# First pair of an attention kernel: low queries of head A on GpSimd, and maxima of four tiles from high halves alone

## The reference

```python
scores = scale * matmul(rotate(q), rotate(k).T)
attn = exp(scores - max(scores)); attn = attn / (sum(attn) + 1e-9)
x = (attn @ v), heads side by side          # 2304 x 512
h = x @ w_in                                # 2304 x 1024
solu = h * softmax(h)
out = layer_norm(solu) * g_ln @ w_out       # 2304 x 512
```

## Time and profile before

| | |
|---|---|
| median of 3 runs | 483.8 us (483.62 to 483.8) |
| the profiled execution | 483.53 us |
| its span | 481.8 us |
| PE busy | 473.4 us (98%) |
| DVE, ACT, POOL busy | 381.4, 250.4, 236.1 us |

### The profile page before, as it was taken

How to read it: one execution, slowest core, us unless ns; L and a number is a source line. 1 busy time by engine, 2 the same in 40 slices (tenths; PEclk the granted TensorE clock), 3 DMA queues, 4 the chain that set the end, 5 groups by cost and what they waited for, 6 DMA issues and landing times.

```text
span 481.8 us, 7983 instructions
## 1 busy us (share of the span) xinstructions
PE 473.4 (98%) x2553; PEld 402.9 (84%) x2553; DVE 381.4 (79%) x591; ACT 250.4 (52%) x397; POOL 236.1 (49%) x307
## 2 busy tenths in 40 slices
PE   7899999999999999999999999999999999999997
PEld 7678888988898889888888878888888888888885
DVE  6867898889889888988896366999897899888731
ACT  4667677777777777777777352032223222322221
POOL 6877666867686768667772021342352121222110
PEclk9999999999999999999999999999999999999999
DMA  8503544645455545445424203233333233322242
GB/s 295 188 12 77 151 147 113 184 131 168 101 156 164 161 116 152 145 123 169 135 71 100 68 6 59 34 83 69 85 87 62 51 51 68 80 57 60 59 81 84
DMA packets 101009, 50.61 MB, mean 105 GB/s; under 512 B 90280, under 2 KB 90280, under 8 KB 99048
## 3 DMA queue, kind: packets, MB, share of 16 engines
q1 hardware_dynamic: 100152, 50.00, 38.7%
q10 hardware_dynamic: 816, 0.10, 0.1%
HBM read 33.33 MB, written 4.79 MB: 79 GB/s over the span
## 4 chain that ended last, share of the span: by engine, by line
PE 95%; DVE 2%; ACT 1%; DMA 1%; issue 0%; SPq 0%; DVEq 0%; ACTq 0%
PE ps L1169 20%; PE ps L1183 20%; PE ps L1155 20%; PE ps L1106 18%; PE ps L1077 8%; PE ps L1135 4%; PE ps L1121 4%; DMA X<-x_in 1%; DVE nm L843 1%; DVE X L780 1%; DVE QK L816 0%; DVE X L785 0%; ACT QK L595 0%; ACT p_main L650 0%; ACT QK L610 0%
## 5 line engine op out<-in xcount | busy, mean ns | idle before, releaser
L843 DVE TENSOR_REDUCE nm<-ps 128x1 fp32r<-128x576 f32 x144 | 108.1, 755 | 31.7 <-PE ps L1077 29.1
L1155 PE MATMUL ps<-p_main,V 128*128 128x288 f32 x404 | 114.8, 406 | 0.0
L1169 PE MATMUL ps<-w_hi,KB 128*128 128x512 f32 x288 | 91.5, 390 | 0.0
L1183 PE MATMUL ps<-w_hi,QK 128*128 128x512 f32 x288 | 91.0, 389 | 0.0
L1106 PE MATMUL ps<-QK 128*128 128x288 f32 x320 | 90.0, 362 | 0.8 <-ACT p_main L650 0.5
L650 ACT ACTIVATE p_main<-ps 128x576 f32<-128x576 f32 x101 | 65.7, 651 | 42.6 <-PE ps L1106 41.2
L1155 PEld LDWEIGHTS ps<-p_main,V 128*128 128x128 f32 x404 | 71.0, 190 | 10.8 <-ACT p_main L650 0.2
L412 POOL TENSOR_TENSOR X<-X,rope 128x1152 f32<-128x1152 f32 x26 | 68.5, 2660 | 10.8 <-POOL v_lo_b L453 8.2
L1106 PEld LDWEIGHTS ps<-QK 128*128 128x128 f32 x320 | 55.6, 189 | 17.9 <-issue 5.7
L1106 PE MATMUL ps<-KB 128*128 128x288 f32 x320 | 67.8, 293 | 0.0
L486 POOL COPY V<-oe 32x256 f32<-32x256 f32 x72 | 29.8, 413 | 74.2 <-DVE QK L894 41.6
(11 more groups left out here) (118 smaller groups left out, 717.8 us busy)
## 6 DMA issues: line engine op xcount, KB each, us to landing
X<-x_in SPq DMA_DIRECT2D x13, 1152.0 KB, 5.1
V<-oe SPq DMA_DIRECT2D x213, 32.0 KB, 1.9
V<-v_in SPq DMA_DIRECT2D x32, 160.0 KB, 2.8
out<-X SPq DMA_DIRECT2D x18, 256.0 KB, 2.3
w_raw<-w_in SPq DMA_DIRECT2D x16, 256.0 KB, 2.9
xT<-x_in SPq DMA_DIRECT2D x2, 1152.0 KB, 10.2
xT<-oe SPq DMA_DIRECT2D x16, 144.0 KB, 2.4
inv<-inv_rows SPq DMA_DIRECT2D x16, 144.0 KB, 3.0
```

The costliest lines, as they stand in the source:

```text
L843: nc.vector.tensor_reduce(nm[g][:, at:at + 1], src[:, :, 0:HALF], AX_XY, ALU.max, negate=True)\
L1155: ins = nc.tensor.matmul(o_ps[a][:, half, 0:HALF], v, p[:, half * HALF:(half + 1) * HALF], start=(k == 0), stop=(k == 9))
L1169: ins = nc.tensor.matmul(h_ps[t % 3][:, half, :], left[a][:, c, :], right[:, col:col + 512], start=(c == 0 and k == 0), stop=(c == KC - 1 ...
L1183: ins = nc.tensor.matmul(y_ps[a], left[a][:, c * P:(c + 1) * P], right[:, col:col + 512], start=(i == 0), stop=(i == DOWNS - 1))
```

## The change

The low queries of head A move from DVE's queue to POOL's, ahead of head B's low keys there. On DVE the low keys of head A now stand ahead of the second copy of its high queries, which waits for ACT's high queries too. The first four tiles of maxima are products over head A's own 64 partitions, high queries with high keys, so that they wait for neither the low keys nor the second copy; the fifth tile waits for these in their place.

```diff
@@ gpsimd
             pool.wait_ge(pool_const, 7)
             pool.wait_ge(kb_ones[1], 2)
 
+            pool.wait_ge(hi_done[0], 1)
+            pool.wait_ge(low_k_done[0], 1)
+            low_queries(0, 0)
             pool.wait_ge(first_hi_k[1], 1)
             pool.wait_ge(low_q_done[0], 1)
             low_keys(0, 1)
@@ vector
             def first_second_queries():
 
                 dve.wait_ge(rot_done, 1)
+                dve.wait_ge(hi_done[0], 1)
                 nc.vector.tensor_copy(QK[0][other(0), 0, 0:S], x_of(0)[own(0), 1, :]).then_inc(hi_done[0], 1)
@@ vector
             first_add(0, rot_done)
+            low_keys(0, 0)
             first_second_queries()
-            low_keys(0, 0)
-            low_queries(0, 0)
             dve.wait_ge(pool_const, 7)
@@ tensor, row_scores
-                if i == 0:
+                if i == 0 and m == 0:
+                    pe.wait_ge(hi_done[0], 1)
+                    pe.wait_ge(first_hi_k[0], 1)
+                elif i == 0:
                     pe.wait_ge(hi_done[0], copied(m, 0))
                     if m >= 3:
                         pe.wait_ge(second_done, m - 2)
                         pe.wait_ge(high_k_done[0], m - 2)
                     pe.wait_ge(low_k_done[0], m + 1)
+                    pe.wait_ge(pool_const, 7)
+                if i == BOTH and m == 0:
+                    pe.wait_ge(hi_done[0], 2)
+                    pe.wait_ge(low_k_done[0], 1)
                     pe.wait_ge(pool_const, 7)
                 if i == BOTH:
                     pe.wait_ge(hi_done[1], copied(m, 1))
@@ tensor, row_scores
+                elif m == 0 and i < BOTH:
+                    parts = [(QK[0][own(0), 0, i * P:(i + 1) * P], QK[0][own(0), 1, 0:S])]
                 else:
```

## The result

The changed kernel takes **486.67 us** (median of 6, 485.51 to 488.07) against 483.86 before (median of 6, 483.62 to 484.15): 1.0058 times the time, 95% interval 1.0042 to 1.0074. That is 2.8 us slower, above the 1.0 us that can be told from no change and outside my range (483.6 to 484.9). The profiled execution took 486.77 us, its span 485.0.

What follows compares the result with a forecast made beforehand. TensorE was taken as the bound, with 95% of the chain, so the first score's delay, 16.61 - 16.15 = +0.46 us, carries to the end: 483.8 + 0.46 = 484.3 us, range 483.6 to 484.9.

Steps and rivals of the forecast that it cites:

- Nothing in it changes PE's later work: On PE after the first pair: eight products read 64 rows instead of 128, 288 columns as before; only start times matter.
- (c): On DVE and POOL: both POOL subtractions go ahead of the waiting copy, first maximum 2.2 us later, 486.0 us; chance 0.05.
- The copy goes ahead of POOL: First pair: DVE's second copy starts at 10.86 or 10.87, POOL's first subtraction at 10.90 to 10.95.
- POOL's low queries are held up by the copy: First pair: shared access makes POOL's first subtraction end at 12.58 instead of 12.33, 0.25 us later.
- Rival (b): POOL issues before DVE's second copy, which ends at 12.57; maxima and scores shift +0.68, 484.5 us; chance 0.18.
- Rival (a): DVE's copy leaves POOL alone; head B's low keys end +0.21, scores shift 0.14, 483.9 us; chance 0.17.
- The gap and the second subtraction: On POOL: 0.12 us between its two subtractions, then head B's low keys take 1.41, from 12.70 to 14.11.
- The fifth tile 0.10 behind POOL: On PE: the fifth tile starts at 14.21, 0.10 us after POOL ends head B's low keys at 14.11.
- The change of tile shape is hidden: First pair's maxima: any tile-shape cost is hidden, since a maximum takes 0.67 us and a tile's products 0.47.
- The early start is worth nothing: First maximum starts 0.5 us earlier, but the fifth tile waits for POOL, leaving DVE idle for 0.8 us.
- The shift of the first score: First pair's first score moves from 16.15 to 16.61, +0.46 us.
- A shift of both is carried to the end: A shift of first scores and second pair's data reaches the end, as PE has no idle time behind them; +0.46 us.

Runs made afterwards that it cites:

- rows alone: Kernel before, with only the first four tiles of maxima of the first pair over head A's 64 partitions, waits and queues unchanged: 484.32 us, ratio 1.0013.
- with the old waits: Kernel before with the changed VectorE and GpSimd queues, PE's waits unchanged: 484.42 us; the same plus the 64-row tiles: 486.62 us.
- queues alone: Kernel before with only VectorE's and GpSimd's queues changed, TensorE's 128-row products and waits unchanged: 484.42 us, ratio 1.0016.
- four fillers: Changed kernel plus four unused identity products on TensorE in its idle time ahead of the fifth tile: 484.75 us, ratio 1.0015.
- with both: Kernel before with the changed queues and the four 64-row tiles, but TensorE's original waits: 486.62 us, ratio 1.0042.

## Why the prediction was wrong

**The step that failed** is in its first part: "Nothing in it changes PE's later work", and with it that the sum of the delays is the sum of the time. I read the rows of a product as a matter of its duration ("Half the rows are not half the time") and never as a matter of the clock at which the next products run. The granted clock was in front of me in the earlier trace rows, at 1.00 in each stretch, and I took it for a property of the kernel instead of a quantity that the first pair could lose. None of my rivals had it; (c), the slower one, was a stall on DVE, and didn't happen. The sum gave this term nothing; it measured 2.1 us by the medians and 2.3 in the profiled execution. That it is the clock is shown from both sides: fillers on PE keep it in 20 of 20 executions and the 2.1 us are gone, and rows alone, or two microseconds of idle time alone, take it away with the queues or the rows left as they were.

Point by point for the rest:

- *The copy goes ahead of POOL.* Right: 11.14 and 11.28, 0.14 apart where my bounds left 0.03 to 0.18. Rival (b) didn't occur in any trace that has both. What released POOL was not what I had named: DVE's low keys ended at 11.10, behind ACT's high queries at 11.03, and POOL followed them by 0.18.
- *POOL's low queries are held up by the copy.* Right: 1.58 in place of 1.41, ending 1.27 behind the copy's end (11.59), which is 1.41 less the 0.14 that I had read from L437. The five further traces with this order have 1.26 to 1.28 there. This agrees, up to these 0.14 us, with the Trainium skill's rule that of VectorE in a two-port mode and GpSimd the one that issues first has the shared pair of ports for its whole instruction (SBUF — State Buffer, section "Who interferes with whom"). Rival (a) falls.
- *The gap and the second subtraction.* 0.14 and 1.40, forecast 0.12 and 1.41. Less the 0.26 of the late start POOL was done at 14.14, forecast 14.11.
- *The fifth tile 0.10 behind POOL.* Wrong in the changed kernel, 0.25, and right in the runs with the old waits. I had counted the added waits as free because what they wait for was long there. They make a semaphore instruction more that is worked off only behind the late one.
- *The change of tile shape is hidden.* Right in the changed kernel, where only the fourth tile pays it and DVE sets the pace; not in the run with eight such tiles, where it put the fourth row product back by 0.15.
- *The early start is worth nothing.* Right: 0.97 us of idle time on DVE took it up (forecast 0.8).
- *The shift of the first score:* forecast 0.46, measured 0.66 in the changed kernel, 0.49 with the old waits. In the medians without fallen executions it is 0.56 (queues alone) and 0.74 (four fillers). Of the right kind, 0.15 short for the waits.
- *A shift of both is carried to the end.* Right: constant from the third exponential on, the clock's part too.

What stays open: how TensorE's recent work is weighed for its clock. The runs order the kernels (fallen: 2 of 71 before, 2 of 10 with the queues alone, 6 of 10 with four tiles over 64 rows, 7 of 10 with both, 6 of 6 in the changed kernel, and 4 of 4 both with eight such tiles and with two microseconds of idle time), but two of ten against two of 71 is thin ground for the step from the kernel before to the queues alone. Nor did I try the changed kernel's early first tile over full rows, since the low keys aren't there yet at that time; so what its wait of 1.23 us adds to the rows is open. The changed kernel's step from 7 of 10 to 6 of 6 is within chance. Nor is it shown why some executions of one kernel fall and others don't. The traces show one thing that differs ahead of any changed instruction: the sixty warm-up products start at the same time in all of them and take from 8.30 to 9.81 us. They start 0.21 us apart at first and 0.11 us apart once the clock has risen, and that is at 4.8 us in the trace before and at 6.0 in the changed kernel's.

```profile
1.53 8.52 PE L1039 MATMUL ps<-ident 128*128 128x128 f32 x60 [1.53 <-POOL ident L492]
1.52 9.08 PE L1042 MATMUL ps<-ident 128*128 128x128 f32 x60 [1.52 <-POOL ident L492]
```

The first line is the kernel before, the second the changed one. No run varied this, so that it decides is not shown.

## What to carry to other kernels

Where TensorE is the bound and its work is still thin, at the start or across a stage's seam, count what an edit takes from its activity (rows as well as instructions) beside what it takes from the critical path: here 0.7 us of delay came with 2.1 us of clock. Read the granted clock of the stages around such a spot over several executions, not one; a kernel that keeps it in most may be at the edge. A few useless products in an idle time that is already there cost nothing and kept it here, if they end before the next tile is due.

An earlier start of one engine is worth the latest of the things that its next steps wait for. Move that one first: POOL's two subtractions in the other order, with the second copy on ACT, took away the gap that the change had made.

## What the hardware showed that I had not expected

Products over 64 rows, with the same columns and no less busy time, let TensorE's clock fall from 2.4 to 1.2 GHz: in six of ten executions with eight such products, in four of four with sixteen, against two of 71 with none. A tile's two products then take 0.79 us in place of 0.48. Over the span the mean clock of these executions was 0.988 to 0.996. The six took 0.5 to 3.4 us more than the four of the same kernel with the clock kept, the four 2.3 to 4.0 us more than the kernel before.

A semaphore wait on PE that has long been met can still cost some 0.1 us if it makes one instruction more behind a late one: 0.25 us from POOL's end to the tile with two such instructions, 0.10 with one.
